# Attention into two MLPs on one core: the band mask of the local scores moves from TensorE to VectorE

## What is computed

```python
# attention: batch 4, 8 heads, 576 positions, head size 64
mask = np.abs(pos[:, None] - pos[None, :]) < 4
scores = np.where(mask, scale * q @ k.T, -1e9)
attn = softmax(scores)                 # with the row maximum subtracted
out_local = attn @ v
# q, k, v averaged over groups of 4 positions: a full softmax attention, repeated 4 times
out = out_up + out_local
# first MLP (512 to 2048 to 512) on the 2304 tokens
h = x @ w_in;  x = (h * np.cos(h)) @ w_out
# RMS norm, then the gated second MLP (512 to 1536 to 512)
out = (silu(xn @ w_gate) * (xn @ w_val)) @ w_out2
```

## Time and profile before

| | |
|---|---|
| median of 3 runs | 973.09 us (971.92 to 973.64) |
| the profiled execution | 974.04 us, its span (first to last instruction) 972.3 us |
| PE busy | 951.9 us (98%) in 6104 matmuls |
| DVE, ACT, POOL busy | 591.2, 411.0, 308.9 us |
| DMA | 132.31 MB, mean 136 GB/s |
| granted TensorE clock, mean | 0.999 |

### The profile page before, as it was taken

One profiled execution on the slowest core, in us unless ns is written; L12 is line 12 of the kernel. 1 busy time (PEld: TensorE's weight loads), 2 busy tenths in 40 slices (PEclk: granted clock), 3 DMA queues, 4 the chain that ended last, 5 costly groups with the idle time before them and its releaser, 6 DMA issues.

```text
span 972.3 us, 17493 instructions
## 1 busy us (share of the span) xinstructions
PE 951.9 (98%) x6104; PEld 848.5 (87%) x6104; DVE 591.2 (61%) x1225; ACT 411.0 (42%) x889; POOL 308.9 (32%) x366
## 2 busy tenths in 40 slices
PE   7899999999999999999999999999999999999998
PEld 5678888888888899999989988899899899999997
DVE  6668777776876675675768554445644456544344
ACT  4435445544644454454544433334422234433232
POOL 5948873221422165486474220011200002000000
PEclk9999999999999999999999999999999999999999
DMA  9622211111111134354345665555565555575631
GB/s 290 219 71 99 79 54 54 54 53 54 53 55 53 50 128 150 130 195 169 140 161 185 261 210 148 152 157 159 146 217 151 152 161 162 154 227 162 163 98 65
DMA packets 66173, 132.31 MB, mean 136 GB/s; under 512 B 7088, under 2 KB 7216, under 8 KB 66096
## 3 DMA queue, kind: packets, MB, share of 16 engines
q1 hardware_dynamic: 66096, 131.27, 42.8%
HBM read 104.50 MB, written 26.74 MB: 135 GB/s over the span
## 4 chain that ended last, share of the span: by engine, by line
PE 91%; POOL 3%; DVE 2%; issue 1%; ACT 1%; DMA 1%; SPq 0%; POOLq 0%; ACTq 0%; DVEq 0%
PE ps L1268 28%; PE ps L1270 27%; PE ps L1269 27%; POOL W L519 2%; PE ps L1187 1%; PE ps L1204 1%; PE ps L1342 1%; PE ps L1245 1%; PE ps L1221 1%; PE ps L1237 1%; DMA qk<-qk 1%; PE ps L1224 1%; DVE xs L960 0%; POOL vg_more L493 0%; POOL prob L505 0%
## 5 line engine op out<-in xcount | busy, mean ns | idle before, releaser
L1268 PE MATMUL ps<-xo,wu 128*128 128x384 f32 x504 | 168.7, 335 | 1.5 <-DVE gate_a L1090 1.5
L1269 PE MATMUL ps<-xo,wu 128*128 128x384 f32 x504 | 169.9, 337 | 0.0
L1270 PE MATMUL ps<-xo,wu 128*128 128x384 f32 x504 | 169.4, 336 | 0.0
L1268 PE MATMUL ps<-xs,W 128*128 128x384 f32 x384 | 134.6, 350 | 0.9 <-DVE xs L960 0.9
L1270 PE MATMUL ps<-xs,W 128*128 128x384 f32 x384 | 130.5, 340 | 0.0
L1269 PE MATMUL ps<-xs,W 128*128 128x384 f32 x384 | 130.1, 339 | 0.0
L1268 PE MATMUL ps<-W,ring 128*128 128x512 f32 x288 | 116.4, 404 | 0.1
L1270 PE MATMUL ps<-W,ring 128*128 128x512 f32 x288 | 113.4, 394 | 0.0
L1269 PE MATMUL ps<-W,ring 128*128 128x512 f32 x288 | 113.2, 393 | 0.0
L751 ACT ACTIVATE ub<-ub,consts 128x384 f32<-128x384 f32 x96 | 59.1, 616 | 104.9 <-DVE ub L1049 104.2
L1268 PEld LDWEIGHTS ps<-xo,wu 128*128 128x128 f32 x504 | 94.7, 188 | 8.2 <-DVE gate_a L1090 1.8
(11 more groups left out here) (132 smaller groups left out, 1730.4 us busy)
## 6 DMA issues: line engine op xcount, KB each, us to landing
wu<-wsplit SPq DMA_DIRECT2D x252, 256.0 KB, 2.8
wsplit<-wp SPq DMA_DIRECT2D x84, 256.0 KB, 2.0
W_raw<-w SPq DMA_DIRECT2D x8, 1024.0 KB, 14.6
qk<-qk SPq DMA_DIRECT2D x14, 576.0 KB, 4.2
gv<-wgv SPq DMA_DIRECT2D x12, 512.0 KB, 3.7
vw<-vwin SPq DMA_DIRECT2D x14, 384.0 KB, 3.2
out<-XY SPq DMA_DIRECT2D x18, 256.0 KB, 3.6
vg<-vgrp SPq DMA_DIRECT2D x26, 144.0 KB
```

The source lines that it names most:

```text
L1268: t_.matmul(dst, a_lo, b_hi, start=first, stop=False, skip_group_check=True)
L1269: t_.matmul(dst, a_hi, b_lo, start=False, stop=False, skip_group_check=True)
L1270: return t_.matmul(dst, a_hi, b_hi, start=False, stop=last, skip_group_check=True)
```

## The change

The mask keeps its values but is laid out for all five column blocks, `[128, 5, 64]` in bf16 instead of `[128, 3, 64]`; the bf16 identity goes, and with it its copy. The load of the constants has 128 + 320 columns instead of 128 + 192. On TensorE the three mask matmuls go, and each score matmul starts its own accumulation. On VectorE an addition comes ahead of the maximum: scores (PSUM) plus mask (SBUF) into `prob` (SBUF), with a semaphore of its own, `masked_ready`; the maximum reads `prob` instead of PSUM, and the subtraction reads and writes `prob`. The wait for `pv_done` moves ahead of the addition, and so ahead of the maximum. TensorE's wait for its bank is for `masked_ready` instead of `diff_ready`.

```diff
-    identb = keep("identb", [P, P], BF16)
-    maskb = keep("maskb", [P, 3, WIN], BF16)
+    maskb = keep("maskb", [P, TP, WIN], BF16)
...
-    raw_const = at("raw_const", [P, P + 3 * WIN], F32, xs_at)
+    raw_const = at("raw_const", [P, P + TP * WIN], F32, xs_at)
...
+    masked_ready = sem("masked_ready")
...
-        v.tensor_copy(identb[:, :], raw_const[:, 0:P]).then_inc(setup_dve, 1)
-        v.tensor_copy(maskb[:, :, :].rearrange("p a b -> p (a b)"), raw_const[:, P:P + 3 * WIN]).then_inc(setup_dve, 1)
+        v.tensor_copy(maskb[:, :, :].rearrange("p a b -> p (a b)"), raw_const[:, P:P + TP * WIN]).then_inc(setup_dve, 1)
...
             sl = kind.sl[s].rearrange("p (t k) -> p t k", k=WIN)
+            p = kind.prob[j][:, s, 0:TP, :]
             dve.wait_ge(local_scores, u + 1)
-            v.tensor_reduce(lmax[:, s, :], sl, axis=AX.X, op=ALU.max).then_inc(lmax_ready, 1)
-            dve.wait_ge(lmax_ready, u + 1)
             free = n - kind.lag
             if not (isinstance(free, int) and free < 0):
                 dve.wait_ge(pv_done, free + 1)
-
+            v.tensor_tensor(p, sl, maskb[:, :, :], ALU.add).then_inc(masked_ready, 1)
             v.memset(kind.prob[j][:, s, TP, :], 0.0)
-            v.tensor_tensor(kind.prob[j][:, s, 0:TP, :], sl, lmax[:, s, :].unsqueeze(2).to_broadcast([P, TP, WIN]), ALU.subtract).then_inc(diff_ready, 1)
+            dve.wait_ge(masked_ready, u + 1)
+            v.tensor_reduce(lmax[:, s, :], p, axis=AX.X, op=ALU.max).then_inc(lmax_ready, 1)
+            dve.wait_ge(lmax_ready, u + 1)
+            v.tensor_tensor(p, p, lmax[:, s, :].unsqueeze(2).to_broadcast([P, TP, WIN]), ALU.subtract).then_inc(diff_ready, 1)
...
-                    pe.wait_ge(diff_ready, u)
+                    pe.wait_ge(masked_ready, u)
             elif u > 1:
-                pe.wait_ge(diff_ready, u - 1)
+                pe.wait_ge(masked_ready, u - 1)
...
-            t_.matmul(sl[:, 0:WIN], identb[:, :], maskb[:, 0, :], start=True, stop=False, skip_group_check=True)
-            t_.matmul(sl[:, WIN:(TP - 1) * WIN].rearrange("p (t k) -> p t k", k=WIN), identb[:, :],
-                      maskb[:, 1:2, :].to_broadcast([P, TP - 2, WIN]), start=False, stop=False, skip_group_check=True)
-            t_.matmul(sl[:, (TP - 1) * WIN:TP * WIN], identb[:, :], maskb[:, 2, :], start=False, stop=False, skip_group_check=True)
             for w in range(NW):
                 half, t = w % 2, w // 2
                 ins = t_.matmul(sl[64 * half:64 * half + 64, t * WIN:t * WIN + WIN], q[:, Q0[w]:Q0[w] + WIN], k[:, K0[w]:K0[w] + WIN],
-                                start=False, stop=w >= NW - 2, skip_group_check=True)
+                                start=True, stop=True)
```

More of the change, by code:

```diff
@@ L935, in copy_ptd @@
             v.tensor_copy(kind.probd[j][0:QT, s].rearrange("p a b -> p (a b)"), kind.ptd).then_inc(ptd_copied, 1)
+        dve.wait_ge(setup_dve, 2)
         down_qk(Wide, 0, 0)
@@ L1248, in values @@
             ins.then_inc(pv_done, 1)
-        pe.wait_ge(setup_dve, 3)
+        pe.wait_ge(setup_dve, 2)
         pe.wait_ge(zeroed, 3)
@@ L1481 @@
     gain = inputs["moe2_rms_g"].reshape(KT, P).T
-    const = np.zeros((P, P + 3 * WIN), np.float32)
+    const = np.zeros((P, P + TP * WIN), np.float32)
     const[:, 0:P] = np.eye(P)
     i, j = np.arange(WIN)[:, None], np.arange(WIN)[None, :]
-    for n, t in enumerate((0, 1, TP - 1)):
-        for half in range(2):
-            off = Q0[2 * t + half] - K0[2 * t + half]
-            const[WIN * half:WIN * half + WIN, P + WIN * n:P + WIN * n + WIN] = np.where(abs(i + off - j) < FACTOR, 0.0, NEG)
+    for w in range(NW):
+        t, half = w // 2, w % 2
+        off = Q0[w] - K0[w]
+        const[WIN * half:WIN * half + WIN, P + WIN * t:P + WIN * t + WIN] = np.where(abs(i + off - j) < FACTOR, 0.0, NEG)
     nc = bacc.Bacc("TRN2", target_bir_lowering=False, num_devices=1)
```

## The result

| | before | after |
|---|---|---|
| median | 973.09 us (971.92 to 974.16, 5 runs) | 977.59 us (977.32 to 980.15, 5 runs) |
| ratio | | 1.0058, 95% interval 1.0045 to 1.007 |
| profiled execution, its span | 974.04, 972.3 us | 980.15, 978.4 us |
| PE busy | 951.9 us in 6104 matmuls | 948.4 us in 6008 |
| DVE, POOL busy | 591.2, 308.9 us | 608.2, 312.7 us |

The kernel is slower by 4.5 us between the medians, and by 4.4 to 6.8 us by the interval of the ratio, where no measurable change was forecast. In the new kernel the lines stand up to 6 off: add 900, maximum 903, subtraction 905, q,k averages 875, first score matmul 1185, downsampled scores 1202, the MLP's matmuls 1266 to 1268.

The account below looks back on a forecast made before the run. TensorE was taken to bound batches 1 to 3 and POOL batch 0. Batches 1 to 3 at -1.0 us and batch 0 at +2.3 gave +1.3 on the median 973.09: 974.4 us, range 970.8 to 977.8.

Parts of the forecast that it names:

- the price of VectorE's addition: Softmax of each unit (one head of one pair): the add lengthens VectorE's sequence by 0.46 us, from durations and waits.
- any other engine's instruction is free unless it makes TensorE wait: Batches 1 to 3 inside the first MLP: TensorE is busy 89.9 of the first 90 us, so only its time counts.
- TensorE's saving, 0.16 us per unit: Batches 1 to 3: dropping the mask matmuls saves 0.18 + 0.25 - 0.27 us per unit, 3.8 us over 24 units.
- VectorE's addition in the first pair of a batch: Second hidden tile's first down matmul, without slack: the first unit's 0.46 us falls on TensorE; blocking adds 0.6 in batch 3.
- The exclusion of two SBUF inputs and POOL: The new subtraction and POOL's instructions block each other: 0.6 us in batch 3, and part of batch 0's cost.
- terms (b) and (c): Batch 0: unit 1's longer softmax with half its block, 0.8 us; subtractions of units 2 to 7 holding up POOL, 1.25.
- the case without it: Rival: VectorE and POOL do not block each other; batch 0 costs 0.7, the rest gains 1.6, 972.2 us; chance 0.16.
- Batch 0, +2.3 us, and batch 1, -0.64: Batch 0: longer constants load 0.25, softmax 0.8, POOL held up 1.25; batch 1: 0.30 lost against 0.94 saved.
- the slower rival: VectorE becomes batch 0's chain at the copy of line 935, 3 to 4.5 us there; about 976.5 us; chance 0.29.
- the chain of this stage: Batch 0, 10 to 50 us: POOL, busy 33.4 of 40 us, holds the chain from 15.01 for over 30 us.
- The signs named as proof: Score matmul 0.27 us behind; subtraction 0.43, up to 1.6; down matmul 0.3 to 1 later; transposes of 48.37 2 later.
- the whole saving: Rival: TensorE saves 0.25 us per unit in batches 1 to 3; -2.7 us in all, 970.4 us; chance 0.13.

Follow-up runs that it names:

- e2_pad64: Changed kernel plus 64 semaphore increments that nothing waits for, at the head of VectorE's program; 975.54 us, ratio 1.0033.
- f2_pad64_before: Kernel before plus 64 semaphore increments on VectorE ahead of its wait for the constants; 974.68 us, ratio 1.0019.
- g1_before_pad20: Kernel before plus 20 semaphore increments on VectorE inside its wait for the constants; 977.90 us, ratio 1.0056.
- e1_grow: Kernel before plus one more VectorE memset per unit, of one column that nobody reads; 978.18 us, ratio 1.0063.
- e3_noeps: Changed kernel without VectorE's addition of 1e-9 to the sums; 971.84 us, ratio 0.9994.
- f1_noeps0: Kernel before without VectorE's addition of 1e-9 to the sums; 971.81 us, ratio 0.9993.
- g3_psum_pad64: Changed kernel with the mask added in place in PSUM, maximum and subtraction reading PSUM, plus 64 semaphore increments on VectorE; 974.41 us, ratio 1.0014.
- f3_pad20: Changed kernel plus 20 semaphore increments on VectorE inside its wait for the constants; 977.44 us, ratio 1.0051.
- e4_psum: Changed kernel with the mask added in place in PSUM, maximum and subtraction reading PSUM; 977.65 us, ratio 1.0053.
- f4_noeps_psum: Changed kernel with the mask added in place in PSUM and without the addition of 1e-9 to the sums; 970.64 us, ratio 0.9983.
- g4_bigconst: Kernel before with the constants' load at the changed kernel's length, 128 + 320 columns, the additional ones unused; 972.21 us, ratio 0.9995.

## Why the prediction was wrong

**The step that failed** is the price of VectorE's addition. It was put at durations and waits alone (0.46 us per unit), and what the added instructions do to the place of VectorE's loop in its code was put at nothing, without a reason. The frame "any other engine's instruction is free unless it makes TensorE wait" held: TensorE was made to wait, 1.97 and 2.10 us, by a pause that no term had. There are two turns of the loop, each with 2.5 to 2.6 us of idle VectorE, in front of the one operation that TensorE needs at once. The missing term is 5.3 us by the lengths of batches 2 and 3 (191.47 us together, against 186.17 in e2_pad64). By medians it is 4.4 with the pads (977.59, less 972.34 and the 0.9 of e2_pad64 over f2_pad64_before; 3.6 against the 973.09 of its own comparison), and 5.4 and 5.8 where nothing else was changed (g1_before_pad20, e1_grow). It was not weighed as a rival either. The trace before held the place in plain view (a first reduction with no slack behind the copies of line 1068, in a body of 305 instructions), and the Trainium skill's page above had the size.

**What the terms measured, with the turn quiet.** The sum was +1.3 us; e2_pad64 over f2_pad64_before gives +0.9, and e3_noeps over f1_noeps0 0.0, each by medians with intervals about 1 us wide either way, so that neither is parted from nothing.

- *TensorE's saving, 0.16 us per unit:* right. From the first down matmul of the second hidden tile to the end of the batch, where six units of a batch lie, the kernel before takes 76.22 us and the changed one 75.28 to 75.36: 0.9 us, 0.94 said. The first score matmul stands 0.27 us behind the MLP matmul, as said:

```profile
65.40 0.34 PE L1268 MATMUL ps<-xs,W 128*128 128x384 f32 x1
65.67 0.80 PE L1185 MATMUL ps<-qk 64*64 64x64 f32 x20
```

- *VectorE's addition in the first pair of a batch, +0.46, and +0.6 more in batch 3:* right in kind, somewhat large. That down matmul stands 17.30 and 17.14 us behind the start of batches 2 and 3 in the kernel before, 17.56 and 17.99 in e2_pad64: +0.26 and +0.85, where +0.46 and +1.06 was said. g3_psum_pad64, without the exclusion, has 17.39 and 17.76, so that only about 0.2 in each batch is the exclusion's, where 0.6 in batch 3 alone was said. The batches change from 93.53 and 93.35 us to 92.87 and 93.30, that is -0.7 and 0.0 (rounded), where -0.5 and +0.1 was said.
- *The exclusion of two SBUF inputs and POOL:* it bites. In batch 0 it costs what was said: the first matmul of the first MLP, with which batch 1 begins, stands at 56.93, 56.87 and 59.48 us in f3_pad20, e3_noeps and e2_pad64, and at 55.41, 54.84 and 57.62 in e4_psum, f4_noeps_psum and g3_psum_pad64, their partners without it. That is 1.5 to 2.0 us, where terms (b) and (c) had 1.6 for it. In batches 2 and 3 it is some 0.4 (e2_pad64 against g3_psum_pad64: 92.87 to 92.70, 93.30 to 93.07), 0.6 was said. Yet the medians differ by 1.1 to 1.2 us only, where the forecast and the case without it stood 2.2 apart: batch 1 gives some back (94.04 us in e3_noeps, 95.72 in f4_noeps_psum). By the rule of the Trainium skill cited ahead ("SBUF — State Buffer", "Who interferes with whom") the later of the two blocks each time; the durations up to 1.29 us agree.
- *Batch 0, +2.3 us, and batch 1, -0.64:* batch 0 about right, batch 1 too small. The first MLP begins at 54.7 to 55.0 us in the kernel before, g4_bigconst, e1_grow and g1_before_pad20, and at 56.93 in f3_pad20, the changed kernel without the late first load: +2.0. The other quiet pairs give +2.0 (e2_pad64 over f2_pad64_before, 57.44) and +2.9 (e3_noeps over f1_noeps0, 53.96). Batch 1 is then shorter by 1.1, 1.5 and 1.6 us in these pairs. Why by more than 0.64 is not shown; each is one execution, and the clock's rise moves by several us from one to the next: full-speed matmuls start at 63.1 us in the profiled execution of the kernel before and at 59.4 in g1_before_pad20, whose batch 1 takes 95.89 us instead of 97.70. (The granted-clock column's 1.00 ahead of the rise, which puzzled the prediction, is no reading: the trace's clock records begin with the rise, at 63.06 and 57.71 us.) The chain of waits in the changed kernel's batch 0 no longer stays with POOL but runs over the subtraction and the copy that VectorE owes TensorE, the place named in the slower rival. So the forecast had the chain of this stage wrong and that rival had it right, but not its price: 3 to 4.5 us was said and 2.0 to 2.9 came.

```profile
40.78 0.96 DVE prob L905
41.73 0.38 DVE dmax L911
42.14 0.76 DVE dbias L913
...
45.10 0.37 DVE probd L936
```

- *The signs named as proof:* the 0.27 us, the lengthened subtraction and the later first down matmul came. Where POOL rests, the subtraction takes 0.49 us and not the 0.43 that was said. The transposes of 48.37 came 3.9 us later (52.25), of which 2.0 are the late first load: in f3_pad20 they stand at 50.28, later by the 2 us that was said.

That the time fell within the range is luck: it owes nothing to the range's reasons. By its own sums the slower case ended at +4.2 us, 977.3, and not at the range's 977.8 (as the whole saving, 970.4, lay below the range's 970.8), so that 977.59 lies beyond every case's own sum.

## What to carry to other kernels

Before an instruction is added to a loop of an engine with a long body, count the body with its waits and register instructions, and look in the trace at the turn: whether the engine stands idle there by "issue", and whether an instruction transfer starts between the branch and the first operation behind it. If such a wait appears only after the change, shift the code by some idle instructions, or shorten the body, before judging the change itself: here the same edit reads as +4.5, as +0.9 (both kernels shifted) or as 0 us (both with a shorter body). A comparison of two kernels of different code length should have a partner: the old kernel, with its loop shifted to the new one's place.

## What was not expected of the hardware

- A turn of VectorE's loop that loads its code again costs 2.49 to 2.8 us of that engine, and 5.4 to 5.8 us of the kernel for two turns (g1_before_pad20, e1_grow); 20 instructions that do nothing, outside the loop and in a wait, are enough to bring it about.
- 64 semaphore increments took VectorE 6.3 us, 0.09 us each and one pause of 0.51 (the copy behind them starts at 7.22 us in all four kernels, instead of 2.98 to 3.47): they are no free filling.
- A wait of TensorE of 2 us was followed, in the changed kernel, by a granted clock of 0.50 to 0.57 for 3 to 4 us. The same stands behind both turns in f3_pad20 (0.59 and 0.64 from 160 and 256 us on), behind one of two in e4_psum, and behind none in e1_grow and g1_before_pad20. The three with it have no mask matmuls on TensorE and the two without it have them; whether that is the cause was not tried.
